# Rearranging the start of a fused attention and two-layer feed-forward kernel: first halves together, another unit order, log rows by copies, splits on VectorE

## The chip, the cores and the metric

The kernel runs on one core of one Trainium2 chip. The metric is the time of one execution on the device in microseconds (us), as the median of the runs shown; lower is better. TensorE (PE) multiplies matrices, VectorE (DVE), ScalarE (ACT) and GpSimd (POOL) work elementwise, and SyncE (SP) issues most of the DMAs. Every engine works through its own queue in order, and waits on semaphores.

## What is computed

```python
def _attn_ref(q, k, v, i_gate, f_gate, o_gate):   # B, H, S, D = 2, 8, 768, 40
    for t in range(S):
        m_new = np.maximum(f_gate[:, :, t] + m, i_gate[:, :, t])
        f_stab = np.exp(f_gate[:, :, t] + m - m_new)
        i_stab = np.exp(i_gate[:, :, t] - m_new)
        C = f_stab * C + i_stab * vt kt^T ; n = f_stab * n + i_stab * kt
        y[:, :, t] = sigmoid(o_gate) * (C @ qt) / max(|n . qt|, 1)

def _moe_ref(x, w_gate, w_val, w_out, rms_g):     # x: 1536 x 320, hidden 1536
    xn = x / sqrt(mean(x * x) + 1e-6) * rms_g
    return silu(xn @ w_gate) * (xn @ w_val) @ w_out

def _moe2_ref(x, w_gate, w_val, w_out):
    return sigmoid(x @ w_gate) * (x @ w_val) @ w_out
```

The output is `_moe2_ref(_moe_ref(attention))`, all in float32.

## The kernel before

**Attention.** The recurrence is worked out in chunks of 128 tokens. There are 12 blocks of 128 tokens, t = 0 to 11 (six chunks, two sequences), each in two halves of four heads, so 24 halves j. A half needs an exponent matrix (`exponents`, from the `lhs` and `rhs` rows, which hold the gates' sums of logarithms), its exponential (ScalarE, L531), the scores of q and k (`scores`), their product (VectorE, `weigh_scores`), and the products with v and with the state (`outputs`), which VectorE sums (`combine`). After two halves a block is normalised (`normalise`), its mean square is taken, GpSimd takes the root (`root`), ScalarE scales it (`scale_y`), TensorE turns it (`turn_x`), and ScalarE and VectorE write it as a rounded part and a rest (`round_x`, `rest_x`): `x_hi` and `x_lo`. The state is updated once a block (`state_sums`, `update_state`, `stack_state`, and two copies, `spread_state`).

**Splitting.** Products in float32 are made from rounded values and rests. Weights are loaded by SP into two raw buffers each (`load_gv`, `load_wo`), rounded by ScalarE (`round_gv`, `round_wo`); the rests come from VectorE (`rest_gv`, L915, L918) and, for the output weights of the first layer, from GpSimd (`rest_wo`, L440, L442). q and k come three halves at a time into `qk_raw` (`load_group`); ScalarE rounds them, GpSimd takes the rest (`split_qk`, L414), and SP copies the parts with three DMAs a half into `qk_st` (`spread_qk`).

**Log rows.** The gates are scanned in three parts: chunk 0, chunk 1 and chunks 2 to 5 (`PARTS`). Every half then needs its four rows in `rhs`: GpSimd multiplies the log rows by a selection mask for it (`spread_logs`, L402).

**Units.** The two layers are walked in units: one block of 128 hidden features for 512 tokens. A unit is a gate product and a value product (`gate_products`, `value_products`, L1179, eight matmuls each), ScalarE's activation, three VectorE steps (`gate_hidden`, `value_hidden`, `rest_hidden`) and ScalarE's rounding, and the result product (`result_products`, eight matmuls, L1231 to L1240), which stands one unit later. For the first 512 tokens the first 7 feature blocks (`SPLIT`) are taken in units of 256 tokens: units 0 to 6 for tokens 0 to 255, 7 to 13 for tokens 256 to 511, then 14 to 18 for all 512. The other 60 units follow, so 79.

**Order.** All queues are written out by hand from the same tables. In the prelude the first four halves (t = 0 and 1) are worked through one after the other, each with its outputs, mixed with filler matmuls (`keep_clock_up`, L1080). In the loop `HALF_AT` puts a half into units 0 to 7, 9, 11, 13 to 21, 23, and so on, and in such a unit stand the exponents and scores of half j and the outputs of half j - 1. `PREP_AT` puts the preparation of weight block f into a unit. The long part of the log rows (chunks 2 to 5) is worked out in units 0 to 4, by VectorE, GpSimd and ScalarE. Unit u's gate product waits until VectorE has read that of unit u - 1; its value product waits for VectorE's step on the value product before.

## Time and profile before

| | |
|---|---|
| median of 3 runs | 529.41 us (529.06 to 531.64) |
| profiled execution | 530.7 us, its span 528.4 us |
| TensorE busy | 497.8 us (94%), 2575 instructions |
| VectorE busy | 254.8 us (48%), 497 instructions |
| ScalarE busy | 195.7 us (37%) |
| GpSimd busy | 90.1 us (17%) |
| mean granted clock of TensorE | 0.952 |
| chain that ended last | PE 78%, DMA 6%, SP's queue 5%, issue 3%, POOL 3%, DVE 3%, ACT 2% |

The page also gives the span in 40 slices of 13.2 us. Tenths of busy time and of the granted clock in the first 16, then the same to the end:

```profile
PE   7978739988999999999999999999999999999996
PEclk8576966999999999999999999999999999999999
```

A digit of 9 is 90% or more. Only the first eight or so slices show a low clock or much idle time; how long each lasts and what it waits for is read from the stretches and the timeline.

### The profile page before, as it was taken

The numbers are of one execution on the slowest core, as the hardware profiler recorded it, in microseconds if no ns is written. First come the engines' busy times: TensorE is split into PE (matmuls) and PEld (weight loads), VectorE is DVE, ScalarE is ACT, GpSimd is POOL, SyncE is SP. The second block draws the span as 40 slices with busy tenths as digits, with TensorE's granted clock in tenths as the row PEclk, the third lists the DMA queues.
The fourth block names the chain that finished last, engine by engine and source line by source line (L and its number), as shares of the span: only waits on it lengthen the run. The fifth ranks groups of instructions, "written<-read, shape, count | busy, mean of one in ns | idle before, by whom it ended". The sixth has DMA issues, their size and how long they took to land.

```text
span 528.4 us, 7165 instructions
## 1 busy us (share of the span) xinstructions
PE 497.8 (94%) x2575; PEld 414.7 (78%) x2577; DVE 254.8 (48%) x497; ACT 195.7 (37%) x399; POOL 90.1 (17%) x105
## 2 busy tenths in 40 slices
PE   7978739988999999999999999999999999999996
PEld 4738738988988878888888888888888888888884
DVE  4558984767885565453455455322332222323222
ACT  3544543445554353231554356312221222222212
POOL 3357652425462310000000000000000000000000
PEclk8576966999999999999999999999999999999999
DMA  8238852293844230000022320000000000010001
GB/s 207 77 118 229 218 143 89 87 249 106 228 116 135 89 106 2 1 0 0 14 84 86 123 90 30 1 0 0 1 36 15 0 2 0 21 31 0 1 0 51
DMA packets 20149, 36.78 MB, mean 70 GB/s; under 512 B 2610, under 2 KB 11026, under 8 KB 20114
## 3 DMA queue, kind: packets, MB, share of 16 engines
q1 hardware_dynamic: 19666, 36.05, 24.1%
q10 hardware_dynamic: 448, 0.27, 0.3%
q8 instruction: 21, 0.34, 0.3%
q14 instruction: 14, 0.11, 0.1%
HBM read 23.44 MB, written 1.97 MB: 48 GB/s over the span
## 4 chain that ended last, share of the span: by engine, by line
PE 78%; DMA 6%; SPq 5%; issue 3%; POOL 3%; DVE 3%; ACT 2%; POOLq 0%; ACTq 0%; DVEq 0%
PE bank L1179 47%; PE bank L1231 6%; PE bank L1233 6%; PE bank L1232 6%; SPq L271 3%; PE bank L1133 3%; PE bank L1240 3%; PE bank L1239 3%; DMA qk_st<-qk_parts 2%; POOL qk_parts L414 2%; DMA qk_early<-qk 1%; DMA qk_raw<-qk 1%; PE bank L1139 1%; DMA gv_raw<-wgv 1%; PE bank L1104 1%
## 5 line engine op out<-in xcount | busy, mean ns | idle before, releaser
L1179 PE MATMUL bank<-x_hi,gv_split 128*128 128x512 f32 (+1 forms) x790 | 250.1, 385 | 3.5 <-DVE hid L939 2.2
L1179 PE MATMUL bank<-x_lo,gv_split 128*128 128x512 f32 (+1 forms) x474 | 179.1, 380 | 0.0
L1179 PEld LDWEIGHTS bank<-x_hi,gv_split 128*128 128x128 f32 x790 | 148.3, 193 | 33.2 <-issue 3.9
L1179 PEld LDWEIGHTS bank<-x_lo,gv_split 128*128 128x128 f32 x474 | 91.6, 193 | 16.4
L952 DVE TENSOR_TENSOR hid<-hid,bank 128x512 f32<-128x512 f32 x48 | 33.0, 687 | 137.5 <-PE bank L1179 137.5
L605 ACT ACTIVATE hid_hi<-hid 128x512 fp32r<-128x512 f32 (+1 forms) x79 | 46.8, 592 | 128.5 <-DVE hid L952 93.5
L598 ACT ACTIVATE hid<-bank 128x512 f32<-128x512 f32 (+1 forms) x79 | 43.9, 556 | 110.8 <-PE bank L1179 110.8
L959 DVE TENSOR_TENSOR hid_lo<-hid,hid_hi 128x512 fp32r<-128x512 f32 (+1 forms) x79 | 56.3, 713 | 44.6 <-ACT hid_hi L605 44.1
L1231 PE MATMUL bank<-hid_hi,wo_split 128*128 128x512 f32 (+1 forms) x158 | 60.4, 382 | 3.2 <-DVE hid_lo L959 3.2
L1233 PE MATMUL bank<-hid_hi,wo_split 128*128 128x512 f32 (+1 forms) x158 | 58.9, 373 | 0.0
L1232 PE MATMUL bank<-hid_lo,wo_split 128*128 128x512 f32 (+1 forms) x158 | 58.8, 372 | 0.0
L1231 PEld LDWEIGHTS bank<-hid_hi,wo_split 128*128 128x128 f32 x158 | 30.0, 190 | 9.2 <-issue 3.2
L1232 PEld LDWEIGHTS bank<-hid_lo,wo_split 128*128 128x128 f32 x158 | 30.2, 191 | 5.2
L1233 PEld LDWEIGHTS bank<-hid_hi,wo_split 128*128 128x128 f32 x158 | 30.0, 190 | 5.2
L1133 PEld LDWEIGHTS bank<-v_sb,prob 128*128 128x128 f32 x192 | 29.6, 231 | 2.1 <-DVE prob L838 1.2
L1240 PE MATMUL bank<-hid_lo,wo_split 128*128 128x512 f32 (+1 forms) x79 | 29.6, 375 | 0.0
L1239 PE MATMUL bank<-hid_hi,wo_split 128*128 128x512 f32 (+1 forms) x79 | 29.5, 374 | 0.0
L1133 PE MATMUL bank<-v_sb,prob 128*128 128x42 f32 x192 | 29.0, 309 | 0.1
L939 DVE SCALAR_TENSOR_TENSOR hid<-hid,bank 128x512 f32<-128x512 f32 (+1 forms) x31 | 17.3, 559 | 22.7 <-ACT hid L598 22.6
L948 DVE SCALAR_TENSOR_TENSOR hid<-hid,bank 128x512 f32<-128x512 f32 (+1 forms) x31 | 17.5, 565 | 20.9 <-PE bank L1179 20.4
L402 POOL TENSOR_TENSOR rhs<-log_rows,consts 64x512 fp32r<-64x512 f32 x22 | 24.7, 1128 | 0.9 <-PE bank L1104 0.9
L434 POOL TENSOR_TENSOR rstd<-msq,half_pow 128x1 f32<-128x1 f32 x12 | 6.8, 564 | 74.2 <-DVE msq L886 74.2
(113 smaller groups left out, 489.0 us busy)
## 6 DMA issues: line engine op xcount, KB each, us to landing
qk_st<-qk_parts SPq DMA_DIRECT2D x60, 160.0 KB
gv_raw<-wgv SPq DMA_DIRECT2D x24, 384.0 KB, 4.5
wo_raw<-wo SPq DMA_DIRECT2D x24, 160.0 KB, 4.0
qk_raw<-qk SPq DMA_DIRECT2D x6, 480.0 KB, 6.3
v_sb<-v SPq DMA_DIRECT2D x12, 168.0 KB, 5.5
gate<-og SPq DMA_DIRECT2D x12, 160.0 KB, 5.3
k_sb<-k SPq DMA_DIRECT2D x10, 160.0 KB, 4.1
outT<-y_out SPq DMA_DIRECT2D x6, 256.0 KB, 2.0
```

The costliest lines, as they stand in the source:

```text
L402: nc.gpsimd.tensor_tensor(rhs[j % 2][0:ROWS], log_rows[:, c].unsqueeze(1).broadcast_to([ROWS, HG, L]), consts[0:ROWS, at:at + HG].unsqueez ...
L598: ins = nc.scalar.activation(hid[j][:, 0:size], g_ps[:, 0:size], func, scale=0.5 if tanh else 1.0)
L605: nc.scalar.activation(hid_hi[j][:, 0:size], hid[j][:, 0:size], ACT.Copy).then_inc(hi_done, 1)
L952: ins = nc.vector.tensor_tensor(h, h, v_ps[:, 0:size], ALU.mult)
L959: nc.vector.tensor_tensor(hid_lo[j][:, 0:size], hid[j][:, 0:size], hid_hi[j][:, 0:size].bitcast(F32), ALU.subtract).then_inc(lo_done, 1)
L1133: mm = pe.matmul(pv_ps[:, DV * h:DV * h + DV], prob[g][:, h], v_sb[t % 2][:, HG * g + h], start=True, stop=True)
L1179: mm = pe.matmul(ps[:, 0:size], lhs, rhs, start=(i == 0), stop=(i == len(passes) - 1))
L1231: pe.matmul(out, w_hi, hi, start=first, stop=False)
L1232: pe.matmul(out, w_hi, lo, start=False, stop=False)
L1233: mm = pe.matmul(out, w_lo, hi, start=False, stop=last)
L1239: pe.matmul(out, w_end, hi, start=first, stop=False)
L1240: mm = pe.matmul(out, w_end, lo, start=False, stop=last)
```

## The change

The first four halves are computed back to back at the start, with the outputs after all four exponents; the outputs of t and t - 1 of these have places of their own in PSUM, and blocks 0 and 1 are normalised straight from there. The gates' chunk 0 comes by two small DMAs, the rest later and only once, not twice; the mask factors are smaller and copied by ScalarE. `SPLIT` is 8: units 0 to 7 take tokens 0 to 255, 8 to 15 tokens 256 to 511, 16 to 19 all 512, so there are 80 units. `SCORE_AT` puts the exponents and scores of halves 4 to 7 into units 2 to 5, and of 8 on into units 11 to 18, 20 to 22 and so on; a half's outputs stand one unit later, and the block is turned one unit after that. Where this unit is the first of a block of tokens (unit 20), the result product of the unit before and the turn go ahead of the gate product (`late`). Only one selection mask a buffer is written (`select_rows`), in four `rhs` buffers, and for halves from 4 on SP copies the half's log rows into two rows of `rhs` (`load_rows`, two DMAs of 2 KB each). The splits of q and k and the rests of wo move from GpSimd to VectorE, as do the long part's log rows, now in units 6 to 9 and 11. There are two `k_sb` buffers; `y` is gone, its value stands in `gate`. The early q and k share the space of `hid`, `swap` and the second `gv_raw`, so that `load_gv(1)` waits for the early scores. The fillers stand mostly after the four outputs.

```diff
-SPLIT = 7
+SPLIT = 8
...
-HALF_AT = dict(zip([0, 1, 2, 3, 4, 5, 6, 7, 9, 11, 13, 14, 15, 16, 17, 18, 19, 20, 21, 23, 25, 26],
-                   range(FIRST, HALVES + 2)))
-PREP_AT = dict(zip([0, 1, 2, 3, 4, 8, 10, 12, 14, 15], range(2, NF)))
+SCORE_AT = dict(zip([2, 3, 4, 5, 11, 12, 13, 14, 15, 16, 17, 18, 20, 21, 22, 24, 25, 26, 28, 29], range(FIRST, HALVES)))
+OUT_AT = {u + 1: j for u, j in SCORE_AT.items()}
+NORM_AT = {u: j // 2 for u, j in OUT_AT.items() if j % 2}
+TURN_AT = {u + 1: t for u, t in NORM_AT.items()}
+SUM_AT = {0: 0, 2: 1, **{u: t for u, t in NORM_AT.items() if t < NT - B}}
+PREP_AT = {**{f - 2: f for f in range(2, SPLIT)}, **{SPLIT + f - 4: f for f in range(SPLIT, NF)}}
...
-WARM_START, WARM_ROWS, WARM_SLOT, WARM_TURN = 12, 4, 2, 8
+EARLY = 8
+ROUND_AT = {u: (j - FIRST) // GROUP + 1 for u, j in SCORE_AT.items() if (j - FIRST) % GROUP == 1 and j - 1 + GROUP < HALVES}
+WARM = (10, 2, 1, 0, 0, 0, 0, 9, 8, 5, 6)
...
+            def load_rows(j):
+
+                i, c, at = j % 4, j // 2 // B, pattern(j)
+                sp.wait_ge(log_lo_done, part_of(j) + 1)
+                if j < FIRST + 4:
+                    sp.wait_ge(sel_const, i + 1)
+                else:
+                    sp.wait_ge(arg_done, j - 3)
+                for n in range(2):
+                    sp.dma_start(rhs[i][GATES * n + B * H:GATES * n + B * H + 1].bitcast(F32),
+                                 log_rows[GATES * n + at:GATES * n + at + HG, c - 1]).then_inc(rows_in[i], 16)
...
             def load_gv(n):
+                if n == 1:
+                    sp.wait_ge(s_done, FIRST)
...
-            sp.dma_start(fi_row[:], fi_in).then_inc(gates_in, 16)
+            for n in range(2):
+                sp.dma_start(fi_row[B * H * n:B * H * n + B * H, :, 0], fi_in[:, :, 0]).then_inc(gates_in, 16)
             load_early(0)
+            load_gv(0)
             load_early(1)
+            sp.dma_start(fi_row[0:B * H, :, 1:], fi_in[:, :, 1:]).then_inc(gates_rest_in, 16)
             load_v(0)
+            load_v(1)
             load_gate(0)
-            load_k(0)
-            load_gv(0)
+            load_gate(1)
             load_wo(0)
-            load_v(1)
-            load_gate(1)
             load_group(0)
             load_gv(1)
             load_wo(1)
+            load_k(0)
+            for j in range(FIRST, FIRST + 4):
+                load_rows(j)
+            load_gv(2)
+            load_wo(2)
+            spread_qk(FIRST)
             load_k(1)
-            for j in range(FIRST, FIRST + GROUP):
-                spread_qk(j)
-            load_group(1)
             load_v(2)
-            load_gate(2)
-            spread_state(0)
-            for u in range(-1, PART1 + 1):
+            for u in range(PART1 + 1):
                 gv, out = weight_steps(u + 1)
                 for n in gv:
                     load_gv(n)
                 for n in out:
                     load_wo(n)
-                if u not in HALF_AT:
-                    continue
-                slot = HALF_AT[u]
-                t, g = slot // 2, slot % 2
-                if g == 1 and t + 1 < NT:
-                    load_v(t + 1)
-                    load_gate(t + 1)
-                if g == 1 and (slot - 3) // 2 < NT - B:
-                    spread_state((slot - 3) // 2)
-                if g == 0 and t < NT:
-                    load_k(t)
-                if slot + 3 < HALVES:
-                    spread_qk(slot + 3)
-                    m, i = group_of(slot + 3)
-                    if i == 0 and FIRST + GROUP * (m + 1) < HALVES:
-                        load_group(m + 1)
+                if u in OUT_AT:
+                    j = OUT_AT[u]
+                    t, g = j // 2, j % 2
+                    if g == 0 and t + 1 < NT:
+                        load_v(t + 1)
+                if u == 0:
+                    spread_qk(FIRST + 1)
+                    load_group(1)
+                    load_gate(2)
+                if u == 1:
+                    spread_qk(FIRST + 2)
+                    load_gate(3)
+                if u == 10:
+                    load_rows(FIRST + 4)
+                    load_rows(FIRST + 5)
+                if u in SUM_AT:
+                    spread_state(SUM_AT[u])
+                    load_k(SUM_AT[u] + 2)
+                if u in SCORE_AT:
+                    j = SCORE_AT[u]
+                    if FIRST + 6 <= j + 2 < HALVES:
+                        load_rows(j + 2)
+                    if FIRST + GROUP <= j + 2 < HALVES:
+                        spread_qk(j + 2)
+                        m, i = group_of(j + 2)
+                        if i == 0 and FIRST + GROUP * (m + 1) < HALVES:
+                            load_group(m + 1)
+                if u in TURN_AT and TURN_AT[u] + 2 < NT:
+                    load_gate(TURN_AT[u] + 2)
...
+            def select_rows(i):
+                at = C_SEL_A + HG * i
+                pool.wait_ge(arg_done, i + 1)
+                nc.gpsimd.tensor_copy(rhs[i][0:ROWS], consts[0:ROWS, at:at + HG].unsqueeze(2).broadcast_to([ROWS, HG, L])
+                                      ).then_inc(sel_const, 1)
...
+            pool.wait_ge(gains_in, 16)
+            pool.wait_ge(consts_in, 16)
+            pool.wait_ge(im_done, 1)
+            nc.gpsimd.tensor_tensor(gain_tail[:], gain_col[:, 2:3], tail_w, ALU.mult).then_inc(gain_done, 1)
+            pool.wait_ge(gain_done, 1)
             less_m(1)
             keep_logs(1)
+            for i in range(4):
+                select_rows(i)
+            less_log(1)
+            root(0)
+            root(1)
             pool.wait_ge(cols_done, 1)
             weigh_v(0)
             weigh_v(1)
             for u in range(LAST_BLOCK):
+                if u in TURN_AT:
+                    root(TURN_AT[u])
+                if u in SCORE_AT and SCORE_AT[u] % 2 and SCORE_AT[u] // 2 < NT - B:
+                    t = SCORE_AT[u] // 2
+                    if t == B:
+                        pool.wait_ge(cols_done, 2)
+                    if t == 2 * B:
+                        pool.wait_ge(cols_done, 3)
+                    decay_state(t)
+                    weigh_v(t)
...
+            mask_rows(0, 1)
+            mask_columns(0)
             round_logs(0)
             round_a(0)
+            mask_columns(1)
+            mask_columns(2)
+            exponential(0)
+            mask_columns(3)
+            exponential(1)
+            exponential(2)
+            round_gv(0)
+            exponential(3)
+            gate_tanh(0)
+            gate_tanh(1)
             gate_exponentials(0)
+            mask_rows(1, 2)
+            sum_squares(0)
             round_logs(1)
+            sum_squares(1)
             scale_y(0)
+            scale_y(1)
             round_x(0)
             round_x(1)
             round_gv(1)
...
+                late = u in TURN_AT and u in ENDS
+                if late:
+                    scale_y(TURN_AT[u])
+                    round_x(TURN_AT[u])
                 activate(u)
+                if u == 0:
+                    round_qk(0)
+                    round_wo(0)
+                if u in SCORE_AT:
+                    exponential(SCORE_AT[u])
+                if u in TURN_AT and not late:
+                    scale_y(TURN_AT[u])
                 round_hidden(u)
+                if u in SUM_AT:
+                    round_state(SUM_AT[u])
                 gv, out = weight_steps(u)
+                if u == 0:
+                    round_a(1)
+                    gate_exponentials(1)
+                    round_wo(1)
                 for n in gv:
                     round_gv(n)
                 for n in out:
                     round_wo(n)
+                if u in ROUND_AT:
+                    round_qk(ROUND_AT[u])
+                if u in SCORE_AT and SCORE_AT[u] % 2:
+                    gate_tanh(SCORE_AT[u] // 2)
+                if u == 8:
+                    mask_rows(2, CH)
+                if u == 9:
                     round_logs(2)
                     round_a(2)
                     gate_exponentials(2)
+                if u in TURN_AT and not late:
+                    round_x(TURN_AT[u])
+                if u in NORM_AT:
+                    sum_squares(NORM_AT[u])
...
+            def split_qk(m):
+
+                j = FIRST + GROUP * m
+                n = D * min(GROUP, HALVES - j)
+                dve.wait_ge(qk_rounded, m + 1)
+                if m > 0:
+                    for last in range(j - GROUP, j):
+                        dve.wait_ge(spread_in[last % 4], spread_count(last))
+                nc.vector.tensor_tensor(qk_lo[0:n], qk_raw[0:n], qk_hi[0:n].bitcast(F32),
+                                        ALU.subtract).then_inc(qk_split, 1)
...
             weigh_scores(0)
+            first_spread(3)
+            weigh_scores(1)
+            dve.wait_ge(gates_rest_in, 16)
+            stabiliser(1)
+            weight_rows(0)
+            weigh_scores(2)
+            weigh_scores(3)
+            normalise(0)
             sum_logs(1)
+            normalise(1)
+            mean_square(0)
+            rest_gv(0)
+            mean_square(1)
             rest_logs(1)
+            take_columns(0)
             weight_rows(1)
             rest_x(0)
             rest_x(1)
             rest_gv(1)
             for u in range(UNITS):
+                late = u in TURN_AT and u in ENDS
+                if u in TURN_AT:
+                    mean_square(TURN_AT[u])
+                if late:
+                    rest_x(TURN_AT[u])
                 if u < TANH_UNITS:
                     gate_hidden(u)
+                if u in OUT_AT:
+                    combine(OUT_AT[u])
                 value_hidden(u)
+                if u in SCORE_AT:
+                    weigh_scores(SCORE_AT[u])
+                if u in SUM_AT:
+                    update_state(SUM_AT[u])
+                if u in NORM_AT:
+                    normalise(NORM_AT[u])
                 rest_hidden(u)
+                if u in SUM_AT:
+                    stack_state(SUM_AT[u])
                 gv, out = weight_steps(u)
+                if u == 0:
+                    rest_a(1)
+                    rest_wo(0)
+                    split_qk(0)
+                    decays(1)
+                    rest_wo(1)
+                if u == 1:
+                    take_columns(1)
                 for n in gv:
                     rest_gv(n)
+                for n in out:
+                    rest_wo(n)
+                if u == 6:
+                    stabiliser(2)
+                if u == 8:
+                    last_logs()
+                if u == 9:
                     sum_logs(2)
+                    last_a()
+                    weight_rows(2)
+                if u == 9:
                     rest_logs(2)
                     rest_a(2)
                     decays(2)
+                if u == 11:
                     take_columns(2)
+                if u in ROUND_AT:
+                    split_qk(ROUND_AT[u])
+                if u in TURN_AT and not late:
+                    rest_x(TURN_AT[u])
...
+            keep_clock_up(WARM[0], True)
             early_scores(0)
+            keep_clock_up(WARM[1], True)
             exponents(0)
             exponents(1)
+            keep_clock_up(WARM[2], True)
+            exponents(2)
+            early_scores(1)
+            exponents(3)
+            keep_clock_up(WARM[3], True)
+            outputs(0)
+            keep_clock_up(WARM[4])
+            outputs(1)
+            keep_clock_up(WARM[5])
+            outputs(2)
+            keep_clock_up(WARM[6])
+            outputs(3)
+            keep_clock_up(WARM[7])
+            pe.wait_ge(ident_in, 16)
             turn_gates(0)
+            keep_clock_up(WARM[8])
             turn_x(0)
+            keep_clock_up(WARM[9])
             turn_x(1)
+            keep_clock_up(WARM[10])
             for u in range(UNITS):
+                late = u in TURN_AT and u in ENDS
+                if late:
+                    result_products(u - 1)
+                    turn_x(TURN_AT[u])
                 gate_products(u)
+                if u in SCORE_AT:
+                    exponents(SCORE_AT[u])
+                if u in OUT_AT:
+                    outputs(OUT_AT[u])
+                if u in SUM_AT:
+                    state_sums(SUM_AT[u])
                 value_products(u)
+                if u in SCORE_AT:
+                    scores(SCORE_AT[u])
+                if u > 0 and not late:
+                    result_products(u - 1)
+                if u == 1:
+                    turn_gates(1)
+                if u == 11:
                     turn_gates(2)
+                if u in TURN_AT and not late:
+                    turn_x(TURN_AT[u])
             result_products(UNITS - 1)
```

## Rows read from the trace of the kernel before

**Rows 1.** By stretch: length, each engine's busy us (count), TensorE clock, DMA share, GB/s.

```profile
0.00:37.85 37.85, 30.62 (x137) 19.70 (x139) 19.27 (x50) 15.97 (x39) 14.47 (x28) 0.68 0.51 134
...
37.85:129.81 91.96, 74.14 (x574) 71.69 (x575) 69.53 (x141) 44.36 (x107) 47.83 (x48) 0.85 0.58 159
...
129.81:528.40 398.59, 393.05 (x1868) 323.28 (x1866) 166.03 (x309) 135.33 (x255) 27.78 (x30) 1.00 0.15 43
...
10.00:30.00 20.00, 19.27 (x90) 14.45 (x89) 10.79 (x25) 9.29 (x21) 8.79 (x13) 0.50 0.35 96
```

**Rows 2.** TensorE's waits in the second stretch: total, times, longest.

```profile
PE bank L1104 <- issue: 7.6, 1, 7.6
```

**Rows 3.** Busy time by stretch, around the prelude's gap and its end.

```profile
7.50:10.00 2.50, 0.72 (x10) 0.56 (x8) 1.91 (x6) 0.60 (x3) 0.21 (x1) 0.93 1.05 225
...
30.00:32.50 2.50, 0.61 (x5) 0.28 (x3) 1.46 (x5) 0.94 (x3) 0.20 (x1) 0.97 0.41 128
```

**Rows 4.** Timeline of the prelude: start, length, engine, line, operation; idle before and releaser.

```profile
3.92 0.41 DVE L727 TENSOR_TENSOR_SCAN m_row<-fi_row 32x128 f32<-32x128 f32 x1 [3.92 <-DMA fi_row<-fi_in]
...
9.44 1.90 PE L1113 MATMUL bank<-qk_early 40*128 40x128 f32 x16 [1.78 <-DMA qk_early<-qk]
...
9.79 0.61 POOL L450 CAST rhs<-prob 64x512 fp32r<-64x512 f32 x1 [4.93 <-DMA prob<-masks]
...
24.66 1.77 PE L1133 MATMUL bank<-v_sb,prob 128*128 128x42 f32 x8
```

**Rows 5.** Chain that ended last: start, length, engine and line, count.

```profile
130.92 0.24 PE bank L1104 x2
...
131.16 0.82 PE bank L1133 x8
...
131.97 0.43 PE bank L1139 x4
...
132.40 0.74 PE bank L1153 x16
...
134.28 0.40 PE bank L1123 x4
...
254.94 3.74 PE bank L1179 x16
...
260.50 3.74 PE bank L1179 x16
```

**Rows 6.** Timeline of TensorE: first matmuls of units 8 and 9.

```profile
106.35 0.36 PE L1179 MATMUL bank<-x_hi,gv_split 128*128 128x256 f32 x1
...
109.28 0.28 PE L1179 MATMUL bank<-x_hi,gv_split 128*128 128x256 f32 x1
```

**Rows 7.** Groups from 37 to 130: shapes, count, busy us, mean ns, idle.

```profile
L915 DVE SCALAR_TENSOR_TENSOR gv_split<-gv_raw,gain_col,gv_split 128x256 fp32r<-128x256 f32 x16 | 11.7, 771 | 3.5 <-ACT w_tail L583 3.5
...
L959 DVE TENSOR_TENSOR hid_lo<-hid,hid_hi 128x256 fp32r<-128x256 f32 x12 | 10.1, 845 | 5.2 <-ACT hid_hi L605 5.2
...
L414 POOL TENSOR_TENSOR qk_parts<-qk_raw,qk_parts 120x1024 fp32r<-120x1024 f32 x4 | 9.5, 2371 | 10.2 <-ACT qk_parts L524 10.2
...
L442 POOL TENSOR_TENSOR wo_split<-wo_raw,wo_split 128x256 fp32r<-128x256 f32 x8 | 7.2, 902 | 0.0
...
L838 DVE TENSOR_TENSOR prob<-bank,prob 128x512 f32<-128x512 f32 x10 | 6.9, 687 | 0.3 <-PE bank L1123 0.3
...
L939 DVE SCALAR_TENSOR_TENSOR hid<-hid,bank 128x256 f32<-128x256 f32 x13 | 5.3, 407 | 1.2 <-ACT hid L598 1.1
```

**Rows 8.** Timeline: a VectorE operation of the prelude beside GpSimd's qk split.

```profile
26.84 2.27 DVE L866 TENSOR_SCALAR den<-hsum 128x8 f32<-128x8 f32 x1
```

**Rows 9.** DMA issues, 37.85 to 95: count, KB each, median us to landing.

```profile
gv_raw<-wgv SPq DMA_DIRECT2D x5, 384.0 KB, 6.0
...
wo_raw<-wo SPq DMA_DIRECT2D x5, 160.0 KB, 5.2
```

**Rows 10.** Timeline of SP's queue: a copy inside SBUF.

```profile
53.56 0.76 SPq L307 DMA_DIRECT2D s_st<-s_st  x1
```

493 lines of the change are left out of this document (177 added, 316 removed).

## The prediction

> **What bounds the kernel now.** I read the stretches first: the span falls into three pieces, cut at the first matmul of unit 0 (37.85) and at the first matmul of unit 13 (129.81) [rows 1]. In the last piece TensorE is busy 393.1 of 398.6 us at the full clock: nothing that the change reorders there can give much. The first two pieces last 37.9 and 92.0 us, with a granted clock of 0.68 and 0.85. The waits of TensorE in the second piece [rows 2] come next: 7.6 us in one place, the exponents of half 8, which wait for VectorE's rest of the long a rows. VectorE is busy 69.5 of 92.0 us there, and one TensorE instruction in a unit (a first product) waits for a VectorE instruction of the unit before, so VectorE's queue is what paces this piece, with TensorE's clock falling after each stall.
>
> How much is lost there? At full clock a 256-token unit takes 2.93 us of TensorE (106.35 to 109.28), a 512-token one 5.56 us (254.94 to 260.50), a half 1.89 us (exponents 0.24, outputs 0.82 + 0.43, scores 0.40), a state sum 0.74 [rows 5, 6]; a turn I put at 0.25 and the gate turns at 0.6 together, from their number of matmuls. The loop before holds 14 x 2.93 + 65 x 5.56 + 20 x 1.89 + 9 x 0.74 + 10 x 0.25 + 0.6 = 450 us. Up to unit 13 it holds 61 us (13 units, 10 exponents and scores, 9 outputs, 5 state sums, 4 turns), and takes 92.0: 31 us lost. After it: 398.6 - 389.2 = 9.4 lost, most of it the tail.
>
> **Part 1, the prelude.** The bound from below is the chain of the gates. VectorE's first scan starts at 3.92 [rows 4] and waits for the gates' DMA; the DMA becomes two small ones, and I leave the scan where it is. ScalarE now also copies a mask (0.4) and a column mask (0.6, as GpSimd's copy of it) before the log rows; then rounding, rest and spread give the first exponents at about 8.1. Before, they wait for three copies of GpSimd, the first of which starts at 9.79 [rows 4], as its mask has landed by then. Exponents 1 and 2 follow at 8.7 and 9.5 (VectorE's spreads, 512 elements each), then the second pair's early scores, whose data cannot be much earlier than the 9.44 of before [rows 4], because one weight load of 384 KB is put in front: 10.3. The last exponents end near 12.4, and the four outputs then run one after the other: 1.8 us each at half clock [rows 4], to 19.7. Before, the fourth ends at 26.4 [rows 4], since each output waited for its weighing in turn. Behind them stand 9 + 8 + 5 + 6 filler matmuls instead of 8 + 8: at half clock 28 x 0.43 = 12.0 us, at full clock 6.0. Normalising (1.6), the squares, the root (0.56) and the scaling (0.9) of the second part of the tokens run beside them, from 19.7 to about 24.8, then two turns (0.7 each at half clock), rounding 0.5 and rest 0.56. With the half clock all along, the loop starts at 33.5; with the full clock all along, outputs end at 16.5 and the chain gives 23. Before, the clock falls at 10 after a gap on TensorE (busy 0.72 of 2.5 us), stays at 0.50 for 20 us, and is at 0.97 from 30, right after eight fillers in a row [rows 1, 3]. I take the same: low from 10, full again after the first nine fillers (23.6). Then 8 fillers end at 25.7, the turns at 26.1 and 27.6, x_lo of the second at 28.9. So unit 0 starts at 28.9 instead of 37.9: -9.0 (bounds -4.4 and -15).
>
> **Part 2, units 0 to 15.** Slots 4 to 7 now go to units 2 to 5, slots 8 to 12 to units 11 to 15; units 0, 1 and 6 to 10 carry none; the long log rows go to units 6 to 9. TensorE's content up to the first product of unit 16 is 16 x 2.93 - 0.98 (the last result product comes later) + 9 x 0.64 + 8 x 1.25 + 6 x 0.74 + 3 x 0.25 + 0.6 = 67.5 us. VectorE's content goes by one scale: 0.41 us for 256 elements and 0.69 for 512 [rows 7], so about 0.14 and 0.107 per 100 elements. Sixteen hidden units of three steps: 16 x 1.24 = 19.8. Ten blocks of gv rests, 10 x 1.33 (three operations of 256) = 13.3. Twelve wo rests, new on VectorE: 256 and 64 wide, 12 x 0.6 = 7.2 (the wide one takes GpSimd 0.90). Four qk splits, new there too: no row has 1024 elements on VectorE; the scale gives 1.24, so 5.0 (bounds from the 512-element row, 0.69, to GpSimd's 2.37 each: 2.8 and 9.5). Nine weighings 6.2; eight combines (two of 168) 5.2; four normalisations (two of 320, three of 8) 6.4; six states (two of 336) 5.9; three rests of x (384) 1.7; the log rows with scans and column copies 9.3, of which three operations of 512 are new. Sum 80 us, over TensorE's 67.5: VectorE still paces.
>
> What goes on the other side: beside GpSimd's qk split, 2.37 us, VectorE's operation on 8 elements takes 2.27 us [rows 7, 8], and the mean of hid_lo is 0.845 where its size takes 0.41 [rows 7]. In the piece before I count about 16 us of such inflation (12 x 0.43 for hid_lo, 16 x 0.34 and 8 x 0.42 for the gv rests, the rest in scans and small ones); GpSimd keeps only the decays, the weighing of v and the roots here, so it almost all goes. But 12.2 us of work come over for it. The moves nearly cancel; what is won is less than 4 us of VectorE.
>
> Waits on top of the 80: in unit 0 ScalarE rounds wo block 2, whose load waits on SP for VectorE's rest of block 0 in the same unit. Issue plus 5.2 us to landing [rows 9] is 5.7 us, in which ScalarE stands and the tanh of unit 1 stands behind it; VectorE has 1.5 us of other work: +4.2. In unit 1 the same with gv block 3 (6.0 us to landing), queued on SP behind three copies of 0.8 us: +2. In unit 7 the turn of tokens 384 to 511 is the last thing before unit 8 needs it: +2. In unit 9 the log rows go back and forth between ScalarE and VectorE five times: +1.8. In the nine slotted units and units 6 and 10 one hand-over of about 0.45 each: +5. Together 95 us for a content of 67.5, 27.5 lost instead of 31: -3.5. Bounds: 83, if loads always land in time (80 + 3); and 106, if waits keep the ratio to VectorE's busy time that they have now (92.0 / 69.5 = 1.32, times 80). I take 95, between them, since each wait has a name.
>
> **Part 3, from unit 16.** The content left is 451.2 - 67.5 = 383.7 (16 units of 256 and 64 of 512, and one more state sum in the loop than before). The other losses stay at 9.4. New are two exposed turns. At unit 20 the result products of unit 19 and the turn of t = 7 are put ahead of the first product of block 1: value products end 1.9 us after the outputs, then value 0.7, normalising 1.6, rest 0.7 on VectorE until 4.9, TensorE has work only until 3.7: gap 1.2; after the turn, rounding and rest of x: gap 1.2. At unit 32 the turn of t = 11 comes last before block 2: 1.3. Sum +3.7. Log rows by copies: GpSimd's multiplication for each slot goes; the two copies that replace it are priced nowhere in the trace; the nearest are the 52 KB copies in SBUF, 0.76 us of SP each [rows 10]. They are issued two slots ahead (over 10 us), so I take zero, bound +16 x 1 us (rival 3), and none below. Each moves 2 KB.
>
> **Sum.** 28.9 + 95 + 383.7 + 9.4 + 3.7 = 520.7 of span, against 528.4: -7.7. The profiled execution took 530.7 with 2.3 us around the span, 1.3 over the median of 529.41. So 529.4 - 7.7 = 521.7, say 522.
>
> **Rivals.** (1) The forecast, 516 to 527: 0.42. (2) The loads land in time, and the clock holds through the prelude: unit 0 at 25, 84 us for the stage: 25 + 84 + 396.8 = 505.8 of span, 507 us; anything from 503 to 516. For it: the second gap of the prelude shrinks from 1.8 us to under 1, and less traffic stands ahead of each landing. Against it: the outputs keep TensorE on narrow matmuls, and before the clock did not come back over them. 0.25. (3) SP becomes the bound: slower. A slotted unit now issues 5 copies (3.9 us), in units 12 to 15 also a weight pair (0.9), a state's two copies, k, v and gate every second (1.4): 6.3 us, against 2.4 + 2.4 before. It decides where this, with its waits in between, exceeds the unit's 6.5 us: then spread_qk and the rows come late, and each of 16 slots waits 1 us or more, +16, 538 us. For it: SP stands on the chain of the page already for 5% of the span; against it, slots in 512-token units have 7.5 us, and a slot's copies need 0.76 each only while SP isn't waiting. 0.16 for over 532. A rule speaks for this one: by the Trainium skill (DMA: Bandwidth & Descriptors, Rules for kernel authors) many small transfers should be coalesced, as under 64 KB one pays mostly overhead, and its section Anatomy of one DMA (the GpSimd path) gives about 2 us fixed. No row before shows a 2 KB copy; by that rule a copy issued two slots ahead would still be hidden. (4) The change doesn't do what it says: the prelude is shorter but VectorE's added 12 us come on top without the inflation going (waits at 101 to 106 us): 528 to 533. 0.17.
>
> **How the numbers follow.** 0.5% is about what a measurement of this kernel can tell from no change: 526.8 and 532.1. Faster 0.67 (forecast and rival 2), same 0.17 (rival 4), slower 0.16. The range leaves out the far half of rival 2 and of rival 3: 506 to 534.
>
> **What would show it.** The first product of unit 0 at 27 to 31, and a low granted clock from 10 to about 24. First product of unit 16 at 118 to 130, with VectorE busy near 80 us between. No VectorE operation of 2 us. A stall of ScalarE on wo_raw in unit 0 of about 4 us. Gaps on TensorE at units 20 and 32, 2.4 and 1.3. The wait of 7.6 us gone, something smaller in unit 9 or 10. Wrong it would be if TensorE waits for the rows' copies, or if unit 16 comes before 113 or after 132.

## The result, and the profile after

The changed kernel takes 539.7 us (median of 4 runs, 538.76 to 541.04), where the kernel before takes 530.5 on the same chip: a ratio of 1.0166, 95% interval 1.011 to 1.0223. I had forecast 522 us and a range of 506 to 534. It is slower, and the time lies outside the range. Its profiled execution took 539.07 us, with a span of 537.3. Now and then an execution of a kernel is over 1.5% slower than the fastest of the same kernel; such runs are left out of every ratio below, but not out of the medians.

First the stretches, cut where my sum was cut: at the first product of unit 0 and at that of unit 16. The columns are those of [rows 1]: length, then busy us of TensorE, its weight loads, VectorE, ScalarE and GpSimd, the granted clock, the DMA engines' share, GB/s.

```profile
0.00:27.62 27.62, 24.37 (x121) 14.79 (x122) 15.17 (x40) 14.79 (x36) 8.87 (x23) 0.81 0.51 124
27.62:138.70 111.08, 84.53 (x646) 80.90 (x646) 71.57 (x183) 50.13 (x123) 9.10 (x12) 0.83 0.51 140
138.70:537.30 398.60, 389.83 (x1840) 317.82 (x1839) 165.82 (x310) 134.54 (x251) 9.51 (x15) 1.00 0.14 44
```

| | forecast | measured | off by |
|---|---|---|---|
| unit 0 starts | 28.9 | 27.62 | -1.3 |
| units 0 to 15 | 95 (83 to 106) | 111.1 | +16.1 |
| from unit 16 to the end | 396.8 | 398.6 | +1.8 |
| span | 520.7 | 537.3 | +16.6 |

The whole miss lies in the middle line. TensorE's content there is 67.5 us at full clock by the prediction's count; it is busy for 84.5, so by that count 17.0 us are the price of the low clock, and it stands for 26.6. That is 43.6 us lost, where I had put 27.5 and where the kernel before lost 31 in its stage. The page's slices show it too: the clock line is lower for longer than the one of before.

```profile
PE   7976787795998899999999999999999999999996
PEclk9685797999899999999999999999999999999999
```

What TensorE stood for, in units 0 to 15 (total, times, longest), answers to [rows 2]. The wait of 7.6 us is gone, and late scores and turns come instead:

```profile
PE bank L1175 <- ACT prob L524: 7.0, 2, 3.6
PE bank L1207 <- DVE x_lo L946: 6.8, 2, 5.3
PE bank L1233 <- DVE hid L981: 4.9, 2, 2.9
PE bank L1221 <- ACT xn L548: 2.8, 2, 2.1
...
PE bank L1156 <- DMA rhs<-log_rows: 0.3, 1, 0.3
```

The waits come to 26.4 us. In its stage the kernel before had 19.1: beside the 7.6 there were nine more, 11.5 us together, the largest of them this one:

```profile
PE bank L1123 <- ACT prob L531: 3.1, 2, 2.9
```

The first two waits of the changed kernel name ScalarE and VectorE, so the next view is ScalarE's waits in the same units, and with it the moments at which ScalarE stood for a transfer (timeline: start, length, engine, line, operation, in brackets the idle time before and its releaser):

```profile
ACT hid_hi L596 <- DVE hid L990: 25.1, 13, 4.2
ACT gv_split L569 <- DMA swap_raw<-wgv: 7.5, 2, 7.2
...
ACT gv_split L569 <- DMA gv_raw<-wgv: 5.6, 1, 5.6
...
ACT qk_parts L518 <- DMA qk_st<-qk_parts: 3.8, 1, 3.8
```

```profile
45.68 0.51 ACT L569 ACTIVATE gv_split<-swap_raw,gain_col 128x256 fp32r<-128x256 f32 x1 [7.17 <-DMA swap_raw<-wgv]
...
56.70 0.51 ACT L569 ACTIVATE gv_split<-gv_raw,gain_col 128x256 fp32r<-128x256 f32 x1 [5.55 <-DMA gv_raw<-wgv]
...
130.09 1.06 ACT L518 ACTIVATE qk_parts<-qk_raw 120x1024 fp32r<-120x1024 f32 x1 [3.75 <-DMA qk_st<-qk_parts]
```

The 25.1 us for VectorE's product are 13 waits of up to 4.2 us in a chain that begins at TensorE; the longest single waits are those for gv blocks. For these ScalarE stood 1.8 us in the whole stage of the kernel before:

```profile
ACT gv_split L578 <- DMA gv_raw<-wgv: 1.8, 2, 1.5
```

Each of the three long waits has its gap on TensorE, one or two units of work further on, because behind the standing instruction in ScalarE's queue are the next unit's activation, the next exponentials or `round_x`:

```profile
48.23 1.08 PE L1175 MATMUL bank<-qk_st 120*128 120x128 f32 x4 [3.57 <-ACT prob L524]
...
59.26 1.09 PE L1175 MATMUL bank<-qk_st 120*128 120x128 f32 x4 [3.45 <-ACT prob L524]
...
133.02 1.31 PE L1207 MATMUL bank<-vw,k_sb 128*40 128x42 f32 x16 [5.26 <-DVE x_lo L946]
```

Why the blocks came so late is read from SP's queue:

```profile
26.88 0.45 SPq L317 DMA_DIRECT2D gv_raw<-wgv  x1
33.88 0.33 SPq L321 DMA_DIRECT2D wo_raw<-wo  x1
35.02 2.53 SPq L284 DMA_DIRECT2D qk_st<-qk_parts  x3
37.59 0.76 SPq L311 DMA_DIRECT2D k_sb<-k  x1
38.46 1.08 SPq L302 DMA_DIRECT2D v_sb<-v  x1
39.58 0.43 SPq L317 DMA_DIRECT2D swap_raw<-wgv  x1
...
46.36 0.43 SPq L317 DMA_DIRECT2D gv_raw<-wgv  x1
...
59.34 0.33 SPq L317 DMA_DIRECT2D gv_raw<-wgv  x1
```

Between 26.88 and 33.88 SP stands for VectorE's rest of wo block 0, which is a step of unit 0. Behind it wait the spread of q and k, k, v, and gv block 3, asked for at 39.58 and usable at 45.68, 6.1 us later. From 33.88 to 53.35 SP issues nearly without a pause, so that block 4 is asked for at 46.36 only, and it lands later still, at 56.7 (the trace's DMA issues from 46 to 47.2: KB each, us from issue to landing):

```profile
gv_raw<-wgv SPq DMA_DIRECT2D x1, 384.0 KB, 10.3
```

By stretch (columns as above), the DMA engines have little to do right before block 3 is asked for, and little room right after:

```profile
28.00:38.00 10.00, 6.54 (x60) 5.95 (x60) 8.57 (x23) 6.22 (x17) 0.75 (x1) 0.93 0.27 84
38.00:48.00 10.00, 5.46 (x34) 4.81 (x33) 1.70 (x8) 2.74 (x7) 1.49 (x2) 0.50 0.85 209
48.00:58.00 10.00, 7.58 (x42) 7.40 (x42) 3.35 (x9) 2.29 (x7) 0.00 (x0) 0.67 0.88 234
```

In the stretch from 38 to 48 VectorE is busy 1.7 of 10 us, ScalarE 2.7 and TensorE 5.5. What all of them wait for at its end is block 3.

### The profile page after: what moved, and what is told of

It reads as the page before. It is cut to its first block, busy times and chain, and to the rows that moved or that the text cites. A ratio compares the mean times of both kernels' runs of the same rounds, so it can differ in the third digit from the quotient of the medians.

```text
span 537.3 us, 7236 instructions
## 1 busy us (share of the span) xinstructions
PE 498.7 (93%) x2604; PEld 413.5 (77%) x2604; DVE 252.6 (47%) x532; ACT 199.5 (37%) x406; POOL 27.5 (5%) x50
## 4 chain that ended last, share of the span: by engine, by line
PE 81%; issue 9%; DVE 4%; DMA 2%; ACT 2%; SPq 1%; POOL 1%; ACTq 0%; POOLq 0%; DVEq 0%
PE bank L1233 48%; PE bank L1284 6%; PE bank L1285 6%; PE bank L1286 6%; PE bank L1187 3%; PE bank L1293 3%; PE bank L1292 3%; PE bank L1133 2%; PE bank L1207 1%; DMA swap_raw<-qk 1%; PE bank L1175 1%; PE bank L1193 1%; DMA qk_st<-qk_parts 1%; PE bank L1156 1%; PE bank L1221 1%
## 5 line engine op out<-in xcount | busy, mean ns | idle before, releaser
L1233 PEld LDWEIGHTS bank<-x_hi,gv_split 128*128 128x128 f32 x800 | 150.5, 195 | 38.7 <-issue 5.0
L1001 DVE TENSOR_TENSOR hid_lo<-hid,hid_hi 128x512 fp32r<-128x512 f32 (+1 forms) x80 | 51.2, 640 | 38.6 <-ACT hid_hi L596 37.8
L1284 PE MATMUL bank<-hid_hi,wo_split 128*128 128x512 f32 (+1 forms) x160 | 61.8, 386 | 3.5 <-DVE hid_lo L1001 1.9
L1285 PE MATMUL bank<-hid_lo,wo_split 128*128 128x512 f32 (+1 forms) x160 | 60.7, 379 | 0.0
L1286 PE MATMUL bank<-hid_hi,wo_split 128*128 128x512 f32 (+1 forms) x160 | 60.4, 378 | 0.0
L1284 PEld LDWEIGHTS bank<-hid_hi,wo_split 128*128 128x128 f32 x160 | 31.2, 195 | 10.1 <-issue 3.9
L1286 PEld LDWEIGHTS bank<-hid_hi,wo_split 128*128 128x128 f32 x160 | 31.2, 195 | 5.5
L990 DVE SCALAR_TENSOR_TENSOR hid<-hid,bank 128x256 f32<-128x256 f32 (+1 forms) x32 | 17.7, 553 | 26.8 <-PE bank L1233 26.3
L1293 PE MATMUL bank<-hid_lo,wo_split 128*128 128x512 f32 (+1 forms) x80 | 30.2, 377 | 0.0
L1292 PE MATMUL bank<-hid_hi,wo_split 128*128 128x512 f32 (+1 forms) x80 | 30.2, 377 | 0.0
L981 DVE SCALAR_TENSOR_TENSOR hid<-hid,bank 128x256 f32<-128x256 f32 (+1 forms) x32 | 17.6, 550 | 21.8 <-ACT hid L589 21.7
L1187 PEld LDWEIGHTS bank<-v_sb,prob 128*128 128x128 f32 x176 | 23.0, 201 | 0.4
L1187 PE MATMUL bank<-v_sb,prob 128*128 128x42 f32 x176 | 22.8, 282 | 0.0
L1175 PE MATMUL bank<-qk_st 120*128 120x128 f32 x80 | 12.9, 289 | 8.2 <-ACT prob L524 7.4
L1175 PEld LDWEIGHTS bank<-qk_st 120*128 120x128 f32 x80 | 12.5, 210 | 10.4 <-issue 8.5
```

What stands on the lines that cost most here:

```text
L1001: nc.vector.tensor_tensor(hid_lo[j][:, 0:size], hid[j][:, 0:size], hid_hi[j][:, 0:size].bitcast(F32), ALU.subtract).then_inc(lo_done, 1)
L1175: mm = pe.matmul(s_ps(j)[:, L * h:L * h + L], st[:, 1, h], st[:, 0, h], start=True, stop=True)
L1187: mm = pe.matmul(pv_ps(j)[:, DV * h:DV * h + DV], probs(j)[:, h], v_sb[t % 2][:, HG * g + h], start=True, stop=True)
L1233: mm = pe.matmul(ps[:, 0:size], lhs, rhs, start=(i == 0), stop=(i == len(passes) - 1))
L1284: pe.matmul(out, w_hi, hi, start=first, stop=False)
L1285: pe.matmul(out, w_hi, lo, start=False, stop=False)
```

## The experiments

I began with three theories for the 16 us. **S**: supply; ScalarE and VectorE stand in order for weight blocks and spreads that come late, because SP asks for them late. **V**: VectorE's added work sets the pace. **R**: SP is full with the row copies (rival 3 of the prediction). Ratios below are to the kernel before, with 95% intervals. The changed kernel has 1.0166 in its first measurement, and in a second one:

> The changed kernel itself, with nothing edited, timed in the same call as the next two, since runs of one kernel spread over 1%. What it tells is the size of that spread and the base for the comparison: 537 to 541 us, ratio to the kernel before 1.010 to 1.020. Its prelude may end anywhere from 23 to 30 us, by where the clock comes back.

539.55 us, 1.0124 (1.0066 to 1.0183). A difference under 0.5% between two of these kernels tells nothing.

**One load earlier.**

```diff
             load_gv(2)
+            load_gv(3)
             load_wo(2)
```

> Computes everything. One edit to the changed kernel: SP issues the gate/value weight block 3 ahead of the output weight block 2 and the copies of half 4, so it no longer stands behind the wait for VectorE's rest of unit 0. Supply theory (the queue order on SP starves ScalarE, whose stall of 7.2 us before block 3 holds the tanh of unit 2): the stall shrinks to 1 to 3 us, the later one of 5.6 us may move but not grow, 4 to 7 us faster than the changed kernel (530 to 534 of span). Volume theory (the DMA engines are full from 40 to 55 at about 230 GB/s, so order does not matter): the stall moves to another block, within 1 us of the changed kernel (536 to 538 of span).

535.95 us, 1.0054 (1.001 to 1.0098). ScalarE's wait for gv block 3 is gone, and the next two transfers are what it stands for instead; its timeline:

```profile
43.94 0.47 ACT L583 ACTIVATE wo_split<-wo_raw 128x320 fp32r<-128x320 f32 x1 [3.46 <-DMA wo_raw<-wo]
...
51.74 0.51 ACT L571 ACTIVATE gv_split<-gv_raw,gain_col 128x256 fp32r<-128x256 f32 x1 [3.69 <-DMA gv_raw<-wgv]
```

**All early loads forward.** Output blocks 0 and 1 are split in the prelude, so that their raw buffers come free there, and SP asks for blocks 2 and 3 ahead of the row copies.

```diff
             load_k(0)
-            for j in range(FIRST, FIRST + 4):
-                load_rows(j)
+            load_k(1)
             load_gv(2)
             load_wo(2)
+            load_gv(3)
+            load_wo(3)
+            for j in range(FIRST, FIRST + 4):
+                load_rows(j)
             spread_qk(FIRST)
-            load_k(1)
...
+            round_wo(0)
...
+            round_wo(1)
...
+            rest_wo(0)
+            rest_wo(1)
```

> Computes everything. The output weight blocks 0 and 1 are rounded and their rests taken in the prelude instead of unit 0, gate/value block 1 before the last turns, and SP issues weight blocks 2 and 3 and k of t = 1 before the copies of the log rows, into the time from 17 to 27 in which the DMA engines move nothing. Supply theory: TensorE's waits in units 1 to 3 (1.5, 2.0, 1.2, 3.6, 3.5 us) mostly go and with them the half clock from 37 to 53 and 57 to 64: 12 to 18 us faster than the changed kernel, 519 to 525 of span. Volume theory: 3 us at most, from the 10 idle us now used. If VectorE's work is the bound (its 80 us for 16 units), the gain stops at 8 us.

531.45 us, 0.9996 (0.9961 to 1.0031): about half of the miss is won back with the same work on every engine, and units 0 to 15 take 102.8 us in its profile instead of 111.1. This is the largest gain of any single edit, and it speaks for theory S. It isn't the time of asking alone: the steps that free the raw buffers leave unit 0 for the prelude, and ScalarE and VectorE are busy 48.8 and 69.7 us in units 0 to 15 instead of 50.1 and 71.6. Of ScalarE's long waits for blocks one, for block 4, is left in its timeline:

```profile
46.09 0.51 ACT L571 ACTIVATE gv_split<-gv_raw,gain_col 128x256 fp32r<-128x256 f32 x1 [4.53 <-DMA gv_raw<-wgv]
```

**Long log rows spread over units 7 to 10** (`stabiliser(2)` from unit 6 to the end of 7, `rest_a`, `decays`, `round_a` and `gate_exponentials` of part 2 from unit 9 to 10).

```diff
-                if u == 9:
-                    rest_logs(2)
-                    rest_a(2)
+                if u == 9:
+                    rest_logs(2)
+                if u == 10:
+                    rest_a(2)
```

> Computes everything. The long scan of the gates goes from unit 6 to the end of unit 7, behind the last turn that unit 8 needs, and the rounding and rest of the a rows and the gates' exponentials from unit 9 to unit 10. If the two gaps of TensorE before unit 8 (2.1 and 1.2 us, then half clock for 7 us) and the one of 2.9 us before unit 11 come from these steps standing in the queue: gap of 2.1 down to 0.8, the one of 2.9 down to about 1, 3 to 6 us faster than the changed kernel. If the turn's own chain (normalise, square, root, scale) sets unit 8 and ScalarE's steps only move: under 1 us.

536.83 us, 1.011 (1.0074 to 1.0147): at most 3 us, and within what two measurements of one kernel differ by. TensorE's 2.9 us before unit 11 become 2.0 and 1.5, and its 2.1 us for the turn before unit 8 become 0.6. Units 0 to 15 take 110.2 us in its profile, against 111.1 and 110.1 in the two of the changed kernel.

**Rounding q and k a unit later.**

```diff
+                if ROUND_AT.get(u - 1, 0) >= 3:
+                    round_qk(ROUND_AT[u - 1])
...
-                if u in ROUND_AT:
+                if u in ROUND_AT and ROUND_AT[u] < 3:
                     round_qk(ROUND_AT[u])
```

> Computes everything. From the group of halves 13 to 15 on, rounding and splitting of q and k stand one unit later, behind the hidden unit's own steps. In the changed kernel ScalarE stands 3.75 us in unit 14 for the copies of half 12 to land before it may overwrite, and behind it wait the rounding of x, the rest of x, the state sums of unit 15 (5.3 us on TensorE), and then TensorE runs unit 15 at half clock. If that one wait is the cause: 6 to 8 us faster than the changed kernel (529 to 531 of span). If TensorE would wait there for the copies themselves (rows and q, k late on SP): the wait turns up at the exponents or scores of unit 16, and 0 to 2 us.

540.01 us, 1.0156 (1.0085 to 1.0228): nothing won. ScalarE no longer stands in unit 14, and units 0 to 15 take 102.5 us, but TensorE then waits for the spread itself further on, and what follows takes 407.0 us instead of 398.6 (its timeline):

```profile
137.49 1.11 PE L1179 MATMUL bank<-qk_st 120*128 120x128 f32 x4 [5.29 <-DMA qk_st<-qk_parts]
```

**Theory V, by undoing the move.** GpSimd makes the low parts of q and k and of the output weights again.

```diff
-                nc.vector.tensor_tensor(qk_lo[0:n], qk_raw[0:n], ...
+                nc.gpsimd.tensor_tensor(qk_lo[0:n], qk_raw[0:n], ...
```

> One part undone: GpSimd again makes the low parts of q and k (all groups) and of the output weights, VectorE no longer does; all else as in the changed kernel. By my forecast's own account the move is nearly even: 12.2 us of work leave VectorE, inflation by the shared port comes back (hid_lo above 0.43 us, small operations of 2 us), and what is decisive is not VectorE: 538 to 542 us. Rival 1 (VectorE sets the pace, and the move was the mistake): 530 to 536 us. Rival 2 (ScalarE's waits for blocks set the pace, and blocks come free later since GpSimd takes 2.4 us for a split where VectorE takes 1.22): 543 to 548 us, with unit 16 starting 3 us or more later than at 138.7.

546.08 us, 1.0304 (1.0246 to 1.0362): slower still, so the move to VectorE is a gain. As a test of V it is weak: VectorE is busy 69.1 us in units 0 to 15 instead of 71.6, since its other operations get longer (`hid_lo` 0.566 us instead of 0.435). What speaks against V is a run further down, `weights_rows_pool`, with 71.6 us of VectorE's work in 104.5 us of stage instead of 111.1. The loss here is not the one of rival 2 in the expectation. ScalarE's waits for blocks didn't grow (5.6 and 3.6 us); TensorE waits for GpSimd's weighing of v, which is queued behind the split and the spreads that this waits for (TensorE's waits: total, times, longest):

```profile
PE bank L1230 <- POOL vw L449: 12.9, 4, 7.6
```

**Theory R.** The two row copies of a half, from half 8 on, are issued by GpSimd; or, the other way, cut into four on SP.

```diff
-                sp.dma_start(rhs[i][...], log_rows[...]).then_inc(rows_in[i], 16)
+                pool.dma_start(rhs[i][...], log_rows[...]).then_inc(rows_late[i], 16)
```

> The copies of the log rows for the halves from 8 on are issued by GpSimd instead of SP; the four of halves 4 to 7 stay on SP. Nothing else moves. In the changed kernel SP issues without a pause from 111 to 126 and again to 131, some 6.5 us a unit, 1.3 us of it the two row copies of 2 KB, and the spread that unit 14 waits for is issued at 123.9 where unit 13 began at 112.7. Theory A (SP's queue is full in units 12 to 15, which makes the spread late, ScalarE stands 3.75 us and TensorE 5.3 us at 127.8): with 1.3 us a slot less, that wait falls below 2 us and the rest of the slots is not slower: 533 to 537 us. Theory B (the copies are hidden, as I forecast; the stall of unit 15 is due to the DMA traffic, which is the same): 538 to 541 us. If GpSimd's way of issuing costs VectorE more than SP's costs anyone: over 541.

> Each of the two row copies of a half is cut into two copies of 1 KB (two heads each), so four issues on SP instead of two, the same bytes: 1.3 us more of SP per slot, by the 0.65 us that one takes in the changed kernel. Theory A (SP is full in units 12 to 15): those units get 1.3 us longer each, and the wait at unit 15 grows past 8 us: 543 to 548 us, with new waits of TensorE on spreads from unit 16 on. Theory B (the copies are hidden, two slots ahead of their use): 538 to 541 us.

Without them on SP: 535.31 us, 1.0071 (1.0034 to 1.0109), some 4 us better, which is hardly more than two measurements of one kernel differ by. But the wait that theory A named stays, so the gain isn't its; in ScalarE's timeline of that run:

```profile
124.73 1.06 ACT L531 ACTIVATE qk_parts<-qk_raw 120x1024 fp32r<-120x1024 f32 x1 [3.91 <-DMA qk_st<-qk_parts]
```

With four: 541.11 us, 1.0118 (1.0052 to 1.0183, from two runs), not told apart from the changed kernel; theory A's 543 to 548 isn't borne out. The copies cost some 4 us at most, not the 16 of rival 3.

**Spreads a slot earlier.**

```diff
-                    if FIRST + GROUP <= j + 2 < HALVES:
+                    if FIRST + GROUP <= j + 2 < HALVES and group_of(j + 2)[1] == 0:
                         spread_qk(j + 2)
...
+                    if FIRST + GROUP <= j + 3 < HALVES and group_of(j + 3)[1] > 0:
+                        spread_qk(j + 3)
```

> In the changed kernel the spreads of a half that is not the first of its group of three are issued three slots ahead instead of two, as soon as the output four halves back is done; the loads, the rounding and everything else stay. In the changed kernel ScalarE's rounding of the group of halves 13 to 15, in unit 14, stands 3.75 us for the spread of half 12, with round_x and the activation of unit 15 behind it, and TensorE stands 5.3 us at 127.8. Theory A (the spread is simply issued too late, one slot before ScalarE wants it): the spread is issued one unit earlier, ScalarE's wait and TensorE's 5.3 us go, 534 to 536 us. Theory B (what is short is the room in the DMA engines and on SP, so something else is late by as much): 538 to 541 us, with a wait of 3 to 5 us between units 12 and 16 elsewhere.

539.25 us, 1.0118 (1.0059 to 1.0178): nothing won, and theory B has it. ScalarE's 3.75 us are gone; in their place a weight block is late in unit 6, and the row copies, now behind two spreads, are late in unit 14. TensorE's timeline:

```profile
78.84 1.31 PE L1209 MATMUL bank<-vw,k_sb 128*40 128x42 f32 x16 [5.87 <-DVE x_lo L948]
...
126.72 0.80 PE L1158 MATMUL bank<-rhs,lhs 128*128 128x256 f32 x2 [5.08 <-DMA rhs<-log_rows]
```

**Order or room?** Two runs take them apart. In one GpSimd issues the loads of blocks 3 to 11, so that they don't stand in SP's order. In the other the order stays, and the kernel leaves out half of each of these blocks: half of the bytes go, the products are as many.

```diff
-                sp.dma_start(gv_raw[n % 2], ...).then_inc(gv_in[n % 2], 16)
+                pool.dma_start(gv_raw[n % 2], ...).then_inc(gv_soft[n % 2], 16)
```

> In the changed kernel the loads of weight blocks 3 to 11 (gate/value and output) are issued by GpSimd, at the head of the unit before the one that rounds them, instead of by SP, where they stand behind the copies of the attention and the waits of these. Nothing else moves. Theory A (the loads are late because they are queued on SP behind waits for work of other engines): ScalarE's waits for blocks 3 and 4 (7.2 and 5.6 us) shrink by 3 us or more each, SP has 0.9 us less in units 12 to 15, and unit 16 starts 5 to 9 us earlier against unit 0: 531 to 535 us. Theory B (the loads are late because a raw buffer comes free late and landing takes 5 to 6 us): the block is asked for at most a us sooner: 537 to 541 us.

```diff
+                part = slice(0, 1 if 3 <= n < NF else 2)
-                sp.dma_start(gv_raw[n % 2], ...
+                sp.dma_start(gv_raw[n % 2][:, part], ...
```

> In the changed kernel the loads of weight blocks 3 to 11 bring only half of each block (the gate half of the gate/value block, half of each row of the output block), in packets that stay at 1.5 KB and 640 B; what stands in the raw buffer from an earlier block is used for the rest, so the products are wrong and as many. Same queue, same order, same waits, same number of copies; 192 + 80 KB a block less on the DMA engines, which are busy 0.85 to 0.88 of their time from 38 to 58. Theory A (order: the loads are issued late, behind others and their waits): issue times stay, landing shortens by at most 1 to 1.5 us: 536 to 540 us, unit 3 still starts some 13 us after unit 2. Theory B (room: too many bytes are wanted from 38 to 58, since units 2 to 5 now carry both a half and a weight block each in 256-token units): the waits for blocks 3 and 4 lose 3 us or more each, and unit 14's wait for the spread (3.75) goes: 529 to 534 us.

The order: 533.34 us, 1.0047 (1.0009 to 1.0085). Room: 534.18 us, 1.0027 (0.9982 to 1.0073). Each gives more than half of what `supply` gives, so both theories hold in part. With half of the bytes, the same load is asked for as late as before (12.0 us after the start of unit 0, as in the changed kernel) and usable 2.7 us after it was issued instead of 6.1; ScalarE's waits for blocks 3 and 4 fall from 7.2 and 5.6 us to 3.7 and 3.8. SP's queue and ScalarE's timeline of that run:

```profile
40.50 0.43 SPq L318 DMA_DIRECT2D swap_raw<-wgv  x1
```

```profile
43.16 0.51 ACT L571 ACTIVATE gv_split<-swap_raw,gain_col 128x256 fp32r<-128x256 f32 x1 [3.73 <-DMA swap_raw<-wgv]
```

With GpSimd's queue, ScalarE doesn't stand for a gv block at all, and yet only 6 us are won. What TensorE meets instead is the state sum of unit 2, 5.72 us, for which the profile names no releaser in this run. In `weights_rows_pool` below, with the same loads on GpSimd, the same wait is for k, whose load stayed on SP (its timeline):

```profile
41.34 1.31 PE L1240 MATMUL bank<-vw,k_sb 128*40 128x42 f32 x16 [5.85 <-DMA k_sb<-k]
```

**Together.** Do these edits add up?

> The two edits of earlier runs together: the loads pulled forward (531.5 us alone) and the long log rows spread over more units (536.8 alone). If the two act on different waits (units 0 to 5, units 9 and 10), their gains of 8.2 and 2.9 us on 539.7 add: 528 to 530 us. If the later slots give back what is won early, as the loads of units 9 to 15 then come later against TensorE: 531 to 534 us.

531.38 us, 0.9987 (0.9951 to 1.0022): the log rows give nothing on top of the loads.

> The loads pulled forward (531.5 us alone) and the late row copies issued by GpSimd (535.3 us alone) together. If the first acts on units 0 to 5 and the second on units 11 to 19, their gains of 8.2 and 4.4 us on 539.7 add: 526 to 529 us, a ratio to the kernel before of 0.991 to 0.996. If they win the same time: 530 to 533 us.

532.62 us, 1.0033 (0.9985 to 1.0081): GpSimd's row copies give nothing on top either.

> As the run before it, with the long log rows spread over units 7 to 10 as well. Those rows gave 2.9 us alone and nothing on top of the loads. With SP relieved they may show again: 524 to 527 us; if not, the same as the run beside it within 1 us: 526 to 529 us.

1.001 (0.9964 to 1.0056), median 535.16 us. The three together give nothing more than the loads alone.

> Both row copies (from half 8) and the loads of weight blocks 3 to 11 are issued by GpSimd; nothing is pulled forward. Alone they gave 4.4 and 6.4 us on 539.7. If they act on different waits (blocks 3 and 4 against units 11 to 16): 529 to 531 us, and unit 16 under 100 us after unit 0. If both relieve the same queue in the same units: 532 to 535 us.

531.81 us, 1.0015 (0.9978 to 1.0053), and units 0 to 15 take 104.5 us (from 23.87 to 128.37). Nothing is pulled forward here, and the work on VectorE is that of the changed kernel.

> Four edits of the changed kernel together: the loads pulled forward, the long log rows spread over units 7 to 10, the late row copies issued by GpSimd, the spreads three slots ahead. Alone, the first gave 531.5, the third 535.3, and the fourth is run beside this one; the first two together gave 531.4. If the late spread and SP's queue are what is left in units 11 to 16, some 5 us more go: 524 to 528 us, ratio to the kernel before 0.99. If VectorE or TensorE's low clock sets the pace there once the waits are gone: 529 to 532 us.

538.14 us, 1.011 (1.0046 to 1.0174), where the same kernel without `spread_early` has 1.001: it takes back most of what the other three give.

> All the edits that relieve SP or bring loads forward, and the log rows spread: loads 2 and 3 early on SP, blocks 4 to 11 and the row copies issued by GpSimd. It is the candidate for a time under the kernel before: if ScalarE's last 5.0 us of waiting for gv block 4 (in the run with the row copies on GpSimd, early loads and the log rows apart) goes and nothing takes its place, 526 to 529 us, ratio 0.990 to 0.996. If VectorE's queue takes over, as it did where GpSimd issued the weight loads (ScalarE's waits for VectorE's product grew from 21.0 to 29.4 us when its 13 us of waits for blocks went), 530 to 535 us.

It has no ratio: the two runs that its comparison would rest on took 534.97 and 535.23 us, and these show no gain. The loads of the blocks are now early, the DMA engines are 0.95 busy from 40 to 52, and the spread of the first state, issued from 39.9 on, is what comes late; TensorE's timeline:

```profile
52.90 1.04 PE L1230 MATMUL bank<-s_st,qk_st 120*128 120x42 f32 x4 [9.13 <-DMA s_st<-state]
```

No version beats the kernel before by more than can be measured. Five of them stop at its time; where one late transfer was mended, in the runs looked at above, another had become the last.

## Why the prediction was wrong

**The prelude was right.** Unit 0 starts at 27.62 (28.9 forecast), the clock is at half from about 12.5 to 22.5 (10 to 23.6 forecast). The -9.0 was -10.2. Some of that closeness is luck: the second profile of the same kernel starts unit 0 at 30.40, for which see the last section.

**The tail was right.** The two turns that I had called exposed cost 1.61 + 1.17 at unit 20 and 1.17 at unit 32, 3.95 us for 3.7. (By its own terms the content of the loop is 451.0 us and not 451.2; nothing hangs on it.)

**VectorE's prices were right, its role was not.** The qk split takes 1.217 us (1.24 forecast), a rest of the output weights 0.418 + 0.217 (0.6), `hid_lo` 0.435 where it took 0.845 [rows 7], and the gv rest 0.48 where it took 0.77 [rows 7]. VectorE's groups in units 0 to 15:

```profile
L1001 DVE TENSOR_TENSOR hid_lo<-hid,hid_hi 128x256 fp32r<-128x256 f32 x15 | 6.5, 435 | 3.0 <-ACT hid_hi L596 2.9
...
L873 DVE TENSOR_TENSOR qk_parts<-qk_raw,qk_parts 120x1024 fp32r<-120x1024 f32 x4 | 4.9, 1217 | 3.4 <-ACT qk_parts L518 3.4
...
L973 DVE TENSOR_TENSOR wo_split<-wo_raw,wo_split 128x256 fp32r<-128x256 f32 x11 | 4.6, 418 | 0.0
```

It is busy 71.6 us there, not 80. I took it for the pace of the stage, set 80 us as the base and 15 us of waits on top. It stood for 39.5 of 111.1 us. That reading of the kernel before was weak already: in those 92.0 us TensorE's waits that name VectorE come to 7.5 us, and beside them only the 7.6 us for the long a rows hang on it.

**The step that failed is "Waits on top of the 80".** For the wait of unit 1, I put "+2" for gv block 3 "queued on SP behind three copies"; ScalarE stood 7.2 us and TensorE 3.6. The load of block 4 has no term in my sum; ScalarE stood 5.6 and TensorE 3.5. Unit 14's rounding behind the spread has none; ScalarE stood 3.75 and TensorE 5.3. These three are 12.3 us of TensorE's waits for a term of 2, and the low clock comes behind each. My other named waits were nearer: for the +4.2 of unit 0 TensorE stood 1.5 and 2.0 (though ScalarE stood 1.2 us for wo block 2, not about 4), for the +2 of the turn before unit 8 it stood 2.1 and 1.2, for the +1.8 of the log rows 2.9. I had named the mechanism twice, a load that is late on SP, and let it end after unit 1 each time. But everything in SP's queue behind the wait to 33.88 is asked for late, block 4 too, and where all of it is asked for at once a block takes 10.3 us to land instead of 6.1; the 5 to 6 us that I took from [rows 9] didn't hold there. The turning over of two raw buffers adds little: block 6's load stands 6.0 us for block 4's rest, is issued at 59.34 and lands in 3.7 us, and ScalarE doesn't stand for it. A stretch without slots takes the lag up (the DMA engines' share is 0.06 from 88 to 98), and in units 11 to 15 SP issues without a pause again. My upper bound of 106 was a ratio of waits to busy time taken from the old stage, with its own supply, and no bound.

**The price of the clock was left out as a term.** I had 95 us as VectorE's time, so the clock didn't stand in it. Of the 43.6 us lost 17.0 are TensorE at the low clock, which comes after each of the long waits: 0.50 from 38 to 48, 0.67 from 48 to 58, 0.50 from 133 to 138, behind the wait of 5.3 us.

**Rival 3** named the engine but the wrong cargo. SP does issue without a pause for long stretches, yet TensorE waits 0.3 us in all for row copies, and taking them off SP gave 4 us, not 16. The Trainium skill (DMA: Bandwidth & Descriptors, Rules for kernel authors), with its rule to coalesce small transfers, would have had them as costly; here two copies of 2 KB take 1.3 us of SP's issue, and GpSimd's land a median of 2.3 us after issue (the 32 of `rows_pool`), near the 2 us that the page's Anatomy of one DMA (the GpSimd path) gives. The rule didn't decide.

**Why then slower than before, and not equal?** The runs show it in part. Unit 0 to the end takes 509.7 us of span instead of 490.5. The prelude gives 10.2 us; the old stage's 31 us of losses became 43.6 in a stage cut at another unit. Loads forward, with the splits that free their buffers, give back 8 us, and the kernel is then equal to the one before: about what the prelude had won is still lost again behind it. What remains is the density: halves 4 to 7 stand in units 2 to 5 and halves 8 to 12 in units 11 to 15, one in each, and each such 256-token unit also wants a weight block (544 KB) and the spread, q, k, v and gate of its half. That this density and not one cause is behind the last 10 us is argued from the DMA share of 0.85 and 0.88 and from `half_blocks`; I did not try another spacing of the slots, since a turn must be done before unit 8 and the scores of later halves need the long rows. Also open is the spread in unit 14, for which ScalarE stands 2.5 to 4.0 us in the profiles without the edits of `round_later` and `spread_early`.

## What to carry to other kernels

When work is moved off the start of a kernel, read not only which engine was waited for, but when each transfer of the new order is asked for, and what the asking queue stands for at that moment; an in-order engine that waits for a block hands the lag to all that is queued behind it. Where transfers crowd, count the late asking and the longer landing for every block until a stretch with spare time, not once. And try an edit of when loads are asked for before an edit of the work: here it was worth 8 us together with the steps that free the buffers, more than any other.

## What the runs showed of the hardware

**The prelude ends anywhere between 23 and 30 us, in the same instructions.** Unit 0 starts at 27.62 in the changed kernel's first profile and at 30.40 in its second; kernels with the same prelude gave 23.02 (log rows apart), 24.06 (weight loads by GpSimd) and 29.89 (splits on GpSimd). It goes with the clock: the nine fillers behind the outputs take 2.12 us, 0.24 each, where unit 0 starts at 23.02, and 4.05, 0.45 each, where it starts at 27.62. Unit 0 of the changed kernel moved by 2.8 us between its two profiles, 0.5% of the time; the 7 us between the kernels would be 1.3%.

**The record of the granted clock can miss it.** In the profile with the splits on GpSimd nine fillers take 3.39 us from 21.35, 0.38 each, while the stretch from 20 to 24 is given a clock of 1.00. Nine of the same fillers take 2.12 us in the run with the loads forward, also at 1.00. Here the durations are the better witness. The Trainium skill (TensorE: Matmul & The Clock Gate, Seeing it yourself) says that the traced clock events can't be fully trusted; this trace agrees. TensorE's timelines, first of the one kernel, then of the other:

```profile
21.35 3.39 PE L1156 MATMUL bank<-fill 128*128 128x512 bf16 x9
```

```profile
16.30 2.12 PE L1135 MATMUL bank<-fill 128*128 128x512 bf16 x9
```
